# Gated-delta attention and two MLP layers on one core: the attention's order of work written anew, each engine's round taking operations of up to four pairs of chunks

## The reference

```
k_n = k / (norm(k) + 1e-6)
for t in range(S):
    y[t]   = q[t] @ state                       # state is 48x48 per head, zero at the start
    state += beta[t] * outer(k_n[t], v[t] - k_n[t] @ state)
```

## Time and profile before

| | us |
|---|---|
| three runs | 1102.08 (median), 1098.0, 1103.05 |
| the profiled execution, whole | 1103.11 |
| its span, first to last instruction | 1101.3 |
| PE, PEld, DVE, ACT, POOL busy | 1064.8, 1016.9, 546.3, 398.5, 169.5 |

### The profile page before, as it was taken

The page is one execution under the profiler, slowest core; times in us unless marked ns, Lnnn a source line. Parts: engine busy times, 40 slices in busy tenths (PEclk is TensorE's granted clock), DMA queues, the critical chain, the costliest instruction groups (busy, mean ns, idle before and its releaser), DMA issues.

```text
span 1101.3 us, 23844 instructions
## 1 busy us (share of the span) xinstructions
PE 1064.8 (97%) x10226; PEld 1016.9 (92%) x10226; DVE 546.3 (50%) x1079; ACT 398.5 (36%) x758; POOL 169.5 (15%) x220
## 2 busy tenths in 40 slices
PE   3899999999999899999999999999999999999998
PEld 3688889899898899999999999999999999999998
DVE  6677777777778544341331334375243334434221
ACT  2676666766766523221121112142112212211111
POOL 7334444444432310000000000000000000000000
PEclk9899999999999979999999999999999999999999
DMA  5121222112222013010000000030000010000001
GB/s 128 35 45 37 50 50 50 43 29 50 50 51 49 17 58 115 16 57 1 1 1 1 1 1 1 22 103 22 20 25 22 1 44 23 1 32 12 23 22 43
DMA packets 80871, 37.13 MB, mean 34 GB/s; under 512 B 53320, under 2 KB 79744, under 8 KB 80768
## 3 DMA queue, kind: packets, MB, share of 16 engines
q1 hardware_dynamic: 80768, 35.61, 12.1%
HBM read 30.89 MB, written 7.13 MB: 35 GB/s over the span
## 4 chain that ended last, share of the span: by engine, by line
PE 93%; DVE 4%; issue 1%; ACT 1%; POOL 0%; SPq 0%; DMA 0%; DVEq 0%
PE zb L1229 9%; PE zb L1231 9%; PE zb L1230 9%; PE xb L1229 6%; PE xb L1230 6%; PE xb L1231 6%; PE xb L1361 5%; PE pb L1474 4%; PE cb L1398 4%; PE cb L1414 4%; PE pb L1229 4%; PE pb L1230 4%; PE pb L1231 4%; PE zb L1341 2%; PE cb L1410 2%; PE cb L1373 2%
## 5 line engine op out<-in xcount | busy, mean ns | idle before, releaser
L747 DVE SCALAR_TENSOR_TENSOR hid_l<-zb,hid_h 128x384 fp32r<-128x384 f32 x192 | 107.0, 557 | 375.2 <-ACT hid_h L1055 375.1
L1055 ACT ACTIVATE hid_h<-zb 128x384 fp32r<-128x384 f32 x192 | 94.3, 491 | 511.2 <-PE zb L1231 511.2
L1229 PE MATMUL zb<-act_h,w1h 128*128 128x384 f32 x576 | 193.5, 336 | 0.0
L1231 PE MATMUL zb<-act_h,w1l 128*128 128x384 f32 x576 | 193.2, 335 | 0.0
L1230 PE MATMUL zb<-act_l,w1h 128*128 128x384 f32 x576 | 193.0, 335 | 0.0
L1229 PE MATMUL xb<-w2h,hid_h 128*128 128x384 f32 x384 | 133.7, 348 | 0.4
L1230 PE MATMUL xb<-w2l,hid_h 128*128 128x384 f32 x384 | 128.7, 335 | 0.0
L1231 PE MATMUL xb<-w2h,hid_l 128*128 128x384 f32 x384 | 128.6, 335 | 0.0
L839 DVE CAST_PREDICATED zi<-merge_mask,zb 128x512 f16<-128x512 uint8 x144 | 99.1, 697 | 27.2 <-PE zb L1341 25.6
L1229 PEld LDWEIGHTS zb<-act_h,w1h 128*128 128x128 f32 x576 | 108.5, 188 | 0.5
L1230 PEld LDWEIGHTS zb<-act_l,w1h 128*128 128x128 f32 x576 | 108.5, 188 | 0.0
(11 more groups left out here) (211 smaller groups left out, 1909.2 us busy)
## 6 DMA issues: line engine op xcount, KB each, us to landing
stage<-moe_w_ch SPq DMA_DIRECT2D x24, 384.0 KB, 3.4
kq_t<-q_t SPq DMA_DIRECT2D x24, 256.0 KB, 3.6
k_raw<-k SPq DMA_DIRECT2D x24, 192.0 KB, 3.6
v_in<-v SPq DMA_DIRECT2D x24, 192.0 KB, 3.3
y_mem<-x_sb SPq DMA_DIRECT2D x12, 192.0 KB, 6.7
out<-x_sb SPq DMA_DIRECT2D x12, 192.0 KB
out<-y_mem SPq DMA_DIRECT2D x8, 192.0 KB
stage<-c_dft_s SPq DMA_DIRECT2D x3, 385.0 KB, 3.1
```

What stands on the lines that cost most here:

```text
L747: nc.vector.scalar_tensor_tensor(hid_l[:, f % 2], up_b[f % 2][:, 0:HALF], 0.0, hid_h[:, f % 2], ALU.max, ALU.subtract).then_inc(m_hl, 1)
L1055: nc.scalar.activation(hid_h[:, f % 2], up_b[f % 2][:, 0:HALF], ACT.Relu).then_inc(m_hh, 1)
L1229: nc.tensor.matmul(bank, ah, bh, start=start, stop=False)
L1231: return nc.tensor.matmul(bank, al, bh, start=False, stop=stop)
```

## The change

The stages and their operations are as before; the lists that order them are new.

- **Four pairs a round.** The functions take the pair as an argument and are not tied to the body's number. Body s (now -2 to 10) has on PE: the chain of pair s - 1 from its second `solve` group on, the inversion of pair s from level 1's last part, `gram` and `turn_n` of pair s + 1, then `old_values` and the first `solve` of pair s, level 1 of pair s + 1, and `keys` and the first `gram` of pair s + 2. The other engines' lists are cut at similar places (ACT's and DVE's at level 4 of pair s).
- **No products with the zero state.** For pairs 0 and 1 `old_values`, `right` and the product of queries and state in `output` are left out. `solve` of pair 1 waits for `new_state` of pair 0.
- **Identities later.** DVE sums pair 0's squares right after clearing the states, and writes `ident_h`, `x1`, `x1_t` after `one_over_norms(0)`. Of `zi`, ACT writes the levels 1 and 2 after `keys(0, 1)`, POOL the levels 3 to 6.
- **Longer merged end.** Levels 2 to 6 of pair 11 and the chains of pairs 10 and 11 are written out together with `g`, the six `h`, all six `turn` of batch 0, the steps 0 to 7 and the ends 0 to 6 of the MLP, with the staging of ten parts of the weights. `program` goes on from f = 7. The side products up to there alternate between pb[1] and pb[0].

The core of the diff (function bodies that only got the pair as an argument are left out; lists are shown for PE, and in part for the others):

```diff
-        if half == 0 and 1 <= f <= 3:
+        if n and half == 0 and 1 <= f <= 3:
             out += [("turn", n, 1, f - 1)]
...
-START = [("g", 0)] + [("h", 0, j) for j in range(ST)] + [("turn", 0, 0, k) for k in range(KT)]
+START = [("g", 0)] + [("h", 0, j) for j in range(ST)] + [("turn", 0, half, k) for half in range(2) for k in range(KT)]
+MERGED = 7
...
-    start_b = [pb[1], xb[0], xb[1], pb[0], zb[0], zb[1]]
+    start_b = [pb[1], pb[0]]
...
-                for f in range(FT):
+                for f in range(0 if n or half else MERGED, FT):
...
# POOL
+                if c == 0:
+                    eye = ident[:].unsqueeze(1).to_broadcast([C, H, C])
+                    for lv in range(2, LEVELS):
                         for g in range(2):
+                            nc.gpsimd.tensor_copy(zi[:, lv, g], eye).then_inc(s_zi, 1)
...
+            def gated_keys(c):
+                if outside(c) or c // 2 == NC - 1:
+                    return
+                par = c % 2
+                if c >= 2:
                     for g in range(2):
+                        pool.wait_ge(s_c[g], hop_count(c - 2, 6))
...
+            def body(s):
+                keep_t(s, 1)
+                low(s - 1, 1, 0)
+                keep_t(s, 0)
+                unsolved(s - 1, 0)
+                keep(s, 1)
+                unsolved(s - 1, 1)
+                low(s - 1, 0, 1)
+                low(s - 1, 1, 1)
+                squares(s + 2)
+                gated_keys(s + 1)
+                normalise(s + 2)
+                low(s, 0, 0)
+                keep(s + 1, 0)
...
# DVE
             for st in state:
                 nc.vector.memset(st[:], 0.0).then_inc(s_init, 1)
-            dve.wait_ge(s_ident, 16)
-            eye = ident[:].unsqueeze(1).to_broadcast([C, H, C])
-            for t in (x1, x1_t):
-                for g in range(2):
-                    nc.vector.tensor_copy(t[:, g], eye).then_inc(s_init, 1)
-            nc.vector.tensor_copy(ident_h[:], ident[:]).then_inc(s_init, 1)
-            dve.wait_ge(s_init, INITS)
-            dve.wait_ge(s_const, 48)
+            dve.wait_ge(s_init, 2)
...
+            def right(c, g):
+                if outside(c) or c < 2:
+                    return
...
+            def one_over_norms(c):
...
+                if c == 0:
+                    dve.wait_ge(s_ident, 16)
+                    eye = ident[:].unsqueeze(1).to_broadcast([C, H, C])
+                    nc.vector.tensor_copy(ident_h[:], ident[:]).then_inc(s_init, 1)
+                    for t in (x1, x1_t):
+                        for g in range(2):
+                            nc.vector.tensor_copy(t[:, g], eye).then_inc(s_init, 1)
+            def body(s):
+                solution(s - 1, 1)
+                merge(s, 4, 1)
+                gram(s + 1, 1, 1, 0)
+                gram(s + 1, 1, 1, 1)
+                merge(s, 5, 0)
+                square_sums(s + 2)
+                first(s + 1, 0)
+                merge(s, 5, 1)
+                one_over_norms(s + 2)
+                first(s + 1, 1)
+                new_state(s - 1, 0)
+                new_state(s - 1, 1)
+                merge(s, 6, 0)
+                first_t(s + 1, 0)
+                right(s, 0)
+                merge(s, 6, 1)
+                first_t(s + 1, 1)
+                right(s, 1)
+                merge(s + 1, 1, 0)
+                merge(s + 1, 1, 1)
+                gram(s + 2, 0, 0, 0)
+                gram(s + 2, 0, 0, 1)
...
# ACT
+            def inverse_done():
+                for g in range(2):
+                    act.wait_ge(s_mg[g], LEVELS * NPAIR)
+                act.wait_ge(s_x[0], len(X_USE[0]))
...
+                x_part(s, 4, 1, 0)
+                halve(s + 1, 1)
+                x_part(s, 4, 1, 1)
+                output(s - 1, 0)
+                root(s + 2)
+                output(s - 1, 1)
+                x_part(s, 5, 0, 0)
+                n_turned(s + 1, 0)
...
# PE
+            def output(c, g, part):
...
+                for p in range(2 * part, 2 * part + 2):
+                    if c >= 2:
+                        nc.tensor.matmul(cb[g][:, C * p:C * p + C].rearrange("p (o d) -> p o d", d=DP)[:, :, 0:D],
+                                         kq_t[c % NQ][:, g, p, 1], state[c % 2][:, g, p],
+                                         start=True, stop=False, skip_group_check=True)
...
+            def body(s):
+                solve(s - 1, 1, 0)
+                check_back(s - 1, 0, 1)
+                x_part(s, 1, 1, 0)
+                z_part(s, 2, 0)
+                check_back(s - 1, 1, 0)
+                z_part(s, 2, 1)
+                gram(s + 1, 0, 1)
+                x_part(s, 2, 0, 0)
+                x_part(s, 2, 0, 1)
+                check_back(s - 1, 1, 1)
+                x_part(s, 2, 1, 0)
+                z_part(s, 3, 0)
+                x_part(s, 2, 1, 1)
+                solve(s - 1, 0, 1)
+                z_part(s, 3, 1)
+                gram(s + 1, 1, 0)
+                x_part(s, 3, 0, 0)
+                x_part(s, 3, 0, 1)
+                output(s - 1, 0, 0)
+                x_part(s, 3, 1, 0)
+                z_part(s, 4, 0)
+                x_part(s, 3, 1, 1)
+                solve(s - 1, 1, 1)
+                z_part(s, 4, 1)
+                gram(s + 1, 1, 1)
+                x_part(s, 4, 0, 0)
+                output(s - 1, 0, 1)
+                x_part(s, 4, 0, 1)
+                z_part(s, 5, 0)
+                x_part(s, 4, 1, 0)
+                output(s - 1, 1, 0)
+                x_part(s, 4, 1, 1)
+                z_part(s, 5, 1)
+                turn_n(s + 1, 0)
+                output(s - 1, 1, 1)
+                x_part(s, 5, 0, 0)
+                update(s - 1, 0)
+                update(s - 1, 1)
+                x_part(s, 5, 0, 1)
+                z_part(s, 6, 0)
+                x_part(s, 5, 1, 0)
+                turn_n(s + 1, 1)
+                old_values(s, 0)
+                x_part(s, 5, 1, 1)
+                z_part(s, 6, 1)
+                x_part(s, 6, 0, 0)
+                old_values(s, 1)
+                z_part(s + 1, 1, 0)
+                z_part(s + 1, 1, 1)
+                middle(s, s + 2, 0)
+                middle(s, s + 2, 1)
+                keys(s + 2, 0)
+                keys(s + 2, 1)
+                solve(s, 0, 0)
+                x_part(s, 6, 1, 0)
+                x_part(s + 1, 1, 0, 1)
+                gram(s + 2, 0, 0)
+                check_back(s, 0, 0)
+                x_part(s + 1, 1, 0, 0)
+                x_part(s + 1, 1, 1, 1)
...
# PE, from the merged end
+            side_work(("turn", 0, 1, 1))
+            step(0, 0, 0)
+            side_work(("turn", 0, 1, 2))
+            step(0, 0, 1)
+            check_back(NPAIR - 1, 1, 0)
+            check_back(NPAIR - 1, 1, 1)
+            end(0, 0, 0)
+            step(0, 0, 2)
+            end(0, 0, 1)
+            solve(NPAIR - 1, 1, 1)
+            step(0, 0, 3)
+            end(0, 0, 2)
+            solve(NPAIR - 1, 0, 1)
+            step(0, 0, 4)
+            end(0, 0, 3)
+            output(NPAIR - 1, 1, 0)
+            output(NPAIR - 1, 0, 0)
+            step(0, 0, 5)
```

More of the change, by code:

```diff
@@ new lines, in _ @@
+            for s in BODIES:
+                body(s)
+            low_rank_copies()
+            new_state(NPAIR - 2, 0)
+            merge(NPAIR - 1, 4, 1)
+            solution(NPAIR - 2, 1)
+            staging(("V",))
+            side_work(("g", 0))
+            merge(NPAIR - 1, 5, 0)
+            side_work(("h", 0, 0))
+            merge(NPAIR - 1, 5, 1)
+            side_work(("h", 0, 1))
+            merge(NPAIR - 1, 6, 0)
+            side_work(("h", 0, 2))
+            side_work(("h", 0, 3))
@@ new lines, in _ @@
+            for s in BODIES:
+                body(s)
+            solve(NPAIR - 2, 1, 0)
+            check_back(NPAIR - 2, 0, 1)
+            z_part(NPAIR - 1, 2, 0)
+            x_part(NPAIR - 1, 1, 1, 0)
+            check_back(NPAIR - 2, 1, 0)
+            x_part(NPAIR - 1, 2, 0, 0)
+            z_part(NPAIR - 1, 2, 1)
+            x_part(NPAIR - 1, 2, 0, 1)
+            check_back(NPAIR - 2, 1, 1)
+            x_part(NPAIR - 1, 2, 1, 0)
+            z_part(NPAIR - 1, 3, 0)
+            x_part(NPAIR - 1, 2, 1, 1)
@@ new lines, in _ @@
+            output(NPAIR - 2, 1, 1)
+            x_part(NPAIR - 1, 5, 1, 1)
+            x_part(NPAIR - 1, 6, 0, 0)
+            side_work(("h", 0, 4))
+            side_work(("h", 0, 5))
+            z_part(NPAIR - 1, 6, 1)
+            old_values(NPAIR - 1, 1)
+            solve(NPAIR - 1, 0, 0)
+            side_work(("turn", 0, 0, 0))
+            x_part(NPAIR - 1, 6, 1, 0)
+            side_work(("turn", 0, 0, 1))
+            check_back(NPAIR - 1, 0, 0)
+            side_work(("turn", 0, 0, 2))
```

1210 lines of the change are left out of this document (585 added, 625 removed).

## The result

The changed kernel took 1071.49 us (median of 4 runs, 1070.71 to 1071.62) beside 1102.10 for the kernel before (1098.0 to 1103.05): ratio 0.973, 95% interval 0.9708 to 0.9752, so 2.7% faster. The forecast was 1071.0. The kernel before takes either 1097 to 1099 us, at a mean granted clock of 0.993 or 0.994, or 1102 to 1105 at 0.988 to 0.990 (18 later runs), the profiled execution being of the second kind, so that against the first kind the gain is 26.5 us and not 31. The profiled execution took 1070.7, of which the span is 1068.9; before, the span was 1101.3.

The account below looks back on a forecast made before the run. PE's work and waiting were taken to bound the first 403.8 us. Gains 27.9 + 8.1 + 2.5 less 1.2, 3 and 3 gave 31.3 us, so 1071.8 from 1103.1, forecast as 1071; the likeliest's range was 1062 to 1078.

Parts of the forecast that it names:

- The order of bounds: First 403.8 us: PE, or an order that makes it wait, is the bound; 1.4 us of waiting a round.
- old waiting: Bodies 0 to 9, body 10 and merged end: 14, 4.0 and 9.9 us waiting or crawling, together 27.9.
- Steady round: Bodies 1 to 10: exact fits in the new lists lose 0.3 us a round (bounds 0 and 1.4), 3 us.
- three tight places: Steady round: update(s-1,1) no slack; x_part(s+1,1,0,1) needs a merge ending within 0.1; POOL's list 1.2 us of slack.
- Bodies 1 and 2: Without zero products, 24.2 and 26.0 us of PE work, PE narrowly first; 1.2 us given back (bounds 0 and 4).
- Start: Before body 1: square sums at 5.98 instead of 8.47, body 1 at 54 (bounds 50 and 58), net 2.5 us gained.
- The term for the clock: Start: 10 us at 1.2 GHz before; body 1 at 58 if that stretch comes later or lasts longer.
- Merged end: Body 10 and end: 3 us of waiting where the old has 13.9 (bounds 1 and 12); PE should keep full clock.
- Rounds that keep a stall (1): Rounds: update's hand-over misses, 1.4 us a round instead of 0.3, 11 us: 1082; chance 0.14.
- the end that waits (2): Merged end: late weights or a misplaced step idle PE, 6 us of clock and 4 of waits: 1081; chance 0.13.
- the chain of g = 1 (3): Rounds: 14 hand-overs per pair through cb[1] miss their slots, a round grows by 3.8 to 32: 1106; chance 0.07.
- The shared port (4): Start: DVE's casts and POOL's identities shut each other out, DVE's list 3.3 us later: 1074; chance 0.05.

Follow-up runs that it names:

- the keys first: Changed kernel with SyncE's queue reordered, keys of pair c loaded ahead of the values of pair c - 1: 1067.74 us.
- the unmixed end: Changed kernel with the MLP steps behind the last pair's chain instead of between its links, on PE, ACT and DVE: 1081.81 us.
- the filled start: Changed kernel with 58 unused products of the identity with itself where PE stands idle in the start: 1073.99 us.
- the repeat: The changed kernel itself, unaltered, run and traced again for comparison: 1069.99 us over six runs.
- the hand-over of level 1 bare: Changed kernel with each round's two check_back groups moved from between the products of levels 1 and 2 to behind z_part(s, 2, 1): 1081.99 us.

## Why the prediction was right, and where it was off

**The order of bounds** held. PE's starts, not its busy time, gave the waiting: 1.4 us a round, of which 0.3 was to be kept; 1.6 was gained, 1.1 of it by two fills alone. PE now takes 343.6 us from 52.42 to 396.03, and took 376.4 from 52.0 to 428.36. Of the 32.8, 8.1 are products left out and some 4.5 work that PE does ahead of body 1, both by the prediction's costs; 20.2 is waiting and clock. The prediction had 27.9 of old waiting less 7.2 kept (1.2, 3 and 3), which is 20.7. Undone one at a time, the hand-over, the mixing of the end, the identities and the zero products cost 11.3, 11.1, 4.0 and 3.7 us of span, 30.1 of 32.4.

**That it met the median within 0.5 us is luck in part.** By stage it was off by +2.9 against -1.6, -1.8 and -1.4.

**Steady round.** Off by the size of one term: 0.3 us a round of lost fits, and hardly any was lost. The three tight places all held. Moving 0.94 us of DVE's work was enough to break the first of them in every round, so the place without slack was read rightly; it just held. Each round with `middle` is 1.84 longer than one without and not 1.1 as before, which takes back 1.5 of the gain; why is not shown.

**Bodies 1 and 2** are the step that failed in size: "I give back 1.2 for latency (bounds 0, and 4 ...)". It was 4.7 by the same work (54.9 against 50.2), just outside the bound. I had compared DVE's and ACT's busy time with PE's and found PE first, narrowly, and never laid SyncE's queue beside a shorter round. There a load of keys stood behind one of values whose buffer was still in use. With the keys first the two bodies take 51.8, which is 1.6 over the work, where the prediction had 1.2. So 3.1 of the 3.5 us by which the term was short are the queue's.

**Start.** The square sums came at 6.12 for 5.98, and body 1 1.6 us earlier than predicted. The term for the clock was the loose one: 6.8 us at 1.2 GHz against 10.2 before, and it moves with every edit ahead of it (10.2 with the identities early, none with filling products). The sum carried it only in its bounds.

**Merged end.** 60.6 for 62: waits of 1.6 where 3 were taken. The full clock through it was predicted; that it is worth more than the waits is shown by the unmixed end, about 9 us of clock in 12.4.

**The rivals.** Rounds that keep a stall (1): none did; the end that waits (2): it didn't; the chain of g = 1 (3): rounds of 27.98 leave it no place. The shared port (4) is the one whose evidence I misread. I took DVE's casts as 1.2 us each, from a row of two that took 2.43, and a POOL product of 1.47 us beside the first as a sign against a lock. The row of the second pair, which I had not read, has the true length:

```profile
7.02 1.28 DVE L725 CAST x_t<-ident 128x1024 f16<-128x1024 f32 x2
```

A cast alone takes 0.68 us. The two of 2.43 are one of 1.83 and one of 0.68: the first began 0.19 us behind POOL's product (4.48 to 5.95) and ended 0.55 behind its end. POOL's time was unharmed because it was DVE that stood. The kernel with the identities early repeats it with a cast of 128x128, 0.16 us elsewhere:

```profile
4.76 1.47 POOL L610 TENSOR_TENSOR k_sq<-k_raw 128x768 f32<-128x768 f32 x1 [2.39 <-DMA k_raw<-k]
...
5.01 1.29 DVE L743 CAST ident_h<-ident 128x128 f16<-128x128 f32 x1 [2.53 <-DMA ident<-c_ident]
```

So the trace of before had the lock, and the sentence of the prediction that it speaks against it was wrong. Its price in the start was still next to nothing: POOL's identities ended at 19.2 instead of 17.5, just as the next squares fell due (19.19, not 23.9). Its real place was one I had not looked at, `first` against `gated_keys` in body 2, for 1.4 us there in some runs.

The Trainium skill, "Trainium Kernel Development and Optimization", Performance Expectations, prefers the busy share of LDWEIGHTS to that of matmuls. In the steady round after, it is 26.16 of 27.98, and PE has no wait left by its starts; so some 1.8 us of the 3.1 that this measure promised were never there.

## What to carry to other kernels

On an engine whose instructions are pipelined, read waiting from start to start, and fill each short hand-over with an independent group: the same work in another order was worth 1.1 us in 28. When a round is made lighter, look again at everything that it used to hide, the issue queue first: one load that waits for a buffer holds all behind it. Mix the links of a last chain with dense products, for the clock comes on top of the waits; and before something is moved ahead on one engine, see which other engine's queue stands behind what it is moved past, as a fit without slack is paid in each round. ACT's `root`, which waits for DVE and has other work behind it, was such a place in three of these kernels.

## What the runs showed of the hardware

DVE's masked copy of fp16 (`first`, two inputs) and POOL's product of two fp32 tiles do not run side by side. Where the copy begins 0.11 us or more behind the product, the copy is late: it ends 0.59 us behind the product's end, in body 2 of the changed kernel (1.94 us for 0.72) as in both bodies with the filled start (1.95). Where it begins 0.06 us behind the product, or up to 0.2 ahead of it, the product is late and ends 1.29 us behind the copy's end (2.04 us for 1.48 in the repeat, 1.91 in body 1 of the changed kernel). So which one loses changes between runs of one kernel. DVE's fp32 to fp16 cast of the identity and a POOL product do the same to each other: the cast 1.83 for 0.68 or 1.29 for 0.16 where the product began first, the product 1.93 for 1.48 where the cast did. A merge from PSUM showed none of it: 0.67 to 0.74 us for the 71 of 144 that ran beside POOL's work, 0.67 to 0.75 for all.

The Trainium skill, "SBUF — State Buffer", Who interferes with whom, has the pair of ports that DVE and GpSimd share as an exclusive lock, held for a whole instruction, and gives it to the one that issues first. The rows agree with the lock; with the rule of the first only down to some 0.1 us, as the product of the repeat began 0.06 us ahead in the profile and lost. The measurement that I had set against the lock in the prediction was its winner's.

The clock can cost more than the waits in front of it: some 9 us against 3.5 in the unmixed end. There PE was at 1.2 GHz for 20.5 us, in the start between 0 and 10.2 us (17.1 in the kernel before without zero products), in both behind stretches in which PE idled between small groups; 58 products of no use brought it to none in the start, and body 1 only 1.05 us forward, since what PE waits for there comes from DVE and ACT. With the hand-over of level 1 bare, all rounds did the same work and one alone had 3.4 us at 1.2 GHz in it.
